# Who issues the DRAM writes of a chunk's regrouping: SP or ScalarE

## The chip, the core and the metric

The kernel runs on one core of a Trainium2 chip. The core has TensorE (PE in the profile), VectorE (DVE), ScalarE (ACT), GpSimd (POOL) and SyncE (SP). SP computes nothing here, it issues transfers; its queue is SPq in the profile, and a transfer that ScalarE issues stands under ACTq. The metric is the device time of one execution in microseconds (us).

## The reference

Attention over pooled keys, then two gated networks, one after the other. Cut to what matters:

```python
kv_pool = kv.reshape(B, H // 4, 4, W // 4, 4, C).mean(axis=(2, 4))   # B 2, H 384, W 32, C 128
k = v = kv_pool.reshape(B, -1, C) @ w_sr                             # 768 keys
s = (q @ k.transpose(0, 2, 1)) / sqrt(C)                             # 12288 queries a batch
a = exp(s - s.max(-1)); a /= a.sum(-1) + 1e-9
x = (a @ v).reshape(-1, C)                                           # 24576 tokens
h = x @ w1_in;  x = (h * cos(h)) @ w1_out                            # d_ff 2048
h = x @ w2_in;  out = (h * sigmoid(1.702 * h)) @ w2_out
```

Every product of two fp32 matrices that needs it is made of three fp32r matmuls: each operand is split into an upper part (`_hi`, rounded to fp32r) and a lower part (`_lo`, the rest).

## The kernel before

The 24576 queries are 48 chunks of 512 (`CHUNKS`; `CB` = 24 a batch), a chunk is 4 tiles of 128 queries (`SUB`), so there are 192 tiles. The attention fills the first 580 us or so; the two networks, pipelined with each other, fill the rest and are not touched.

A tile goes like this. PE computes its scores against 768 keys (`score`, lines 691 to 693). DVE takes the negated maximum (L1259, `neg_max`), ACT the exponentials (L1038, `exponentials`, into one of two buffers `probs`), DVE turns them by blocks of 32x32 (L1271, `turn`, which counts up `turned_made`). The tile's block lands in `turned[b][n]`, the chunk's buffer, n = chunk modulo 3 (two buffers `turned`, the third is `turned_last`).

The turned blocks still have to be moved between partitions before PE can use them as the moving operand of the product with the values. That is `regroup(c)`, and the DMA does it, in two ways. Blocks are numbered by the group a of 32 partitions in which they lie. For a = 0 and 1 there are 8 direct transfers from SBUF to SBUF, of 96 KB each (L475). For a = 2 and 3 there are two writes of 384 KB to a DRAM tensor `bounce` (L469), and then, when both have landed (semaphore `bounced`), one read of 768 KB back into `gathered` (L479). ACT (two thirds, L1057) and POOL (one third, L613) then round `gathered` to `probs_t_hi`, POOL subtracts to get the lower part (L601), and PE sums (`sum_upper` L763 and L765, `sum_lower` L775). ACT then copies the sums out (L1064, `store_x1`) and SP writes them to DRAM (L492).

Each engine has one order of instructions, written out by hand in a loop over tile slots s = 0 to 190. In slot s, ACT does the exponentials of tile s + 2 first; `round_probabilities(c, i)` comes in slot 4c + 8 + i (`HI_SLOT` is 8), after the exponentials of tiles 4c + 10 and 4c + 11. In slots with s % 4 == 3 ACT also rounds the queries of a later chunk (L1027, `split_queries`) and stores a chunk's sums (L1064). SP runs over chunks: load the queries of chunk c + 3 (L455), for c < 12 a piece of the second batch's keys (L449), `regroup(c)`, save the inverse sums (L487), save chunk c - 3 (L492). The two loads of raw weights ahead of `regroup(18)` and the ones at c = 31 and 35 are on SP too (L500, L504).

`regroup(c)` begins with waits for `turned_made` (the chunk's four tiles) and, from chunk 3 on, for `values_summed` of chunk c - 3, whose lower parts lie in the same bytes as `gathered`. DVE's `turn` of a chunk's first tile waits for `regrouped` of chunk c - 3, since the direct transfers and the writes read the buffer that it is about to fill.

Of the kernel before, what the change touches and what calls it, by code (L numbers as in the profile page):

```python
# [22 lines left out]
BLK = 32  # L23
# [17 lines left out]
def attention_and_networks(nc, q, kv, w_sr, w1_in, w1_out, w2_in, w2_out, out):  # L41
# [4 lines left out]
    KEYS = (H // R) * (W // R)  # L46
# [388 lines left out]
    with nc.Block() as block:  # L435

        @block.sync
        def _(sp):
# [19 lines left out]
            def regroup(c):  # L458

                b, n = c // CB, c % 3  # L460
                sp.wait_ge(turned_made, (c + 1) * SUB)
                if c >= 3:
                    sp.wait_ge(values_summed, c - 2)
                if c == CB + 1:
                    sp.wait_ge(piece_made, 4)
                dst, src = gathered[b][n], turned[b][n]
                for a in range(DIRECT, GROUPS):
                    at = slice((a - DIRECT) * KEYS, (a - DIRECT + 1) * KEYS)
                    sp.dma_start(  # L469
                        bounce[c][:, :, at].rearrange("f p x -> p f x"),  # L470
                        src[a * BLK:(a + 1) * BLK, :, :, :].rearrange("p f k t -> p f (k t)")
                    ).then_inc(bounced[n], 16)
                for a in range(DIRECT):
                    for f in range(GROUPS):
                        sp.dma_start(flat(dst[f * BLK:(f + 1) * BLK, a]),  # L475
                                     flat(src[a * BLK:(a + 1) * BLK, f])
                                     ).then_inc(regrouped[n], 16)
                sp.wait_ge(bounced[n], BOUNCED * (c // 3 + 1))
                sp.dma_start(dst[:, DIRECT:GROUPS].rearrange("p a k t -> p (a k t)"),  # L479
                             bounce[c].rearrange("f p x -> (f p) x")  # L480
                             ).then_inc(regrouped[n], 16)
# [542 lines left out]
        def _(act):  # L1024
# [35 lines left out]
            def store_x1(c):  # L1060
                act.wait_ge(values_summed, c + 1)
                if c >= 2:
                    act.wait_ge(x1_saved[c % 2], c // 2 * 16)
                nc.scalar.activation(by_tile(x_out[c % 2][:, :], "tokens"),  # L1064
                                     by_tile(x1_ps[c % 2], "groups"), ACT.Copy).then_inc(x1_ready, 1)

            def copy_part(t):

                act.wait_ge(part_pooled, t + 1)
                nc.scalar.activation(pooled_t[:, t * TKEYS:(t + 1) * TKEYS], pool1_ps,  # L1070
                                     ACT.Copy).then_inc(part_copied, 1)
# [57 lines left out]
            for s in range(TILES - 1):  # L1129
                if s + 2 < TILES:  # L1130
                    exponentials(s + 2)
                c, i = divmod(s - HI_SLOT, SUB)
                if c >= 0 and i < (BY_POOL if c < CHUNKS - 2 else PARTS):
                    round_probabilities(c, i)
                if s % SUB == 1:
                    guard_totals(s // SUB)
                if (s + 5) % SUB == 0 and 2 <= (s + 5) // SUB < CHUNKS:
                    split_queries((s + 5) // SUB, q_ps)
                if s >= STORE_SLOT and (s - STORE_SLOT) % SUB == 0:
                    store_x1((s - STORE_SLOT) // SUB)  # L1140
                t, m = divmod(s - POOL_SLOT, POOL_GAP)
                if 0 <= t < HT and m == POOL_SLOTS:
                    copy_part(t)
                if s in KEY_SLOTS:
                    key_piece(KEY_SLOTS[s])
                if (s - SPLIT_SLOT) % SPLIT_GAP == 0:
                    i = (s - SPLIT_SLOT) // SPLIT_GAP
                    if 0 <= i < WEIGHT_PIECES:
                        round_weights(i)
            store_x1(CHUNKS - 4)  # L1150
            nc.scalar.activation(silu_probe[:, :], half_pi[:, :], ACT.Silu)
            round_probabilities(CHUNKS - 2, 0)
# [327 lines left out]
```

## Time and profile before

| what | value |
|---|---|
| time, median of 3 runs | 2680.96 us (2680.41 to 2684.88) |
| the profiled execution, its own time | 2679.44 us |
| its span, first to last instruction | 2677.7 us |
| what lies around the span | 1.7 us |
| attention, from the start | about 580 us |
| span from SP's read back of chunk 0 to that of chunk 47 | 41.38 to 572.93 us |

The page gives busy time of each engine over the whole span (PE 97%), the DMA queues and the chain of work that ended last. Since the attention is a fifth of the span, its limits don't show in the shares of the whole; they are read from stretches of it. All transfers of the attention are on one queue, q1, SP's; q10 is ScalarE's, and holds only two stores at the very end.

### The profile page before, as it was taken

What the parts mean: (1) busy time and instruction counts of PE and PEld (TensorE: products, weight loads), DVE (VectorE), ACT (ScalarE), POOL (GpSimd) and SP (SyncE); (2) the same over time, 40 slices, a digit from 0 to 9 for tenths busy, and PEclk for the clock granted to TensorE, in tenths of its full rate; (3) what the DMA queues carried; (4) which work ended last, traced back from release to release, by engine and by line L of the source; (5) the groups of instructions that cost most, each with busy time, mean ns of one, the idle gap of its engine ahead of it and who ended that gap; (6) DMA issues with size and microseconds to landing.
All of it is one profiled execution on the core that took longest, in us unless ns stands there. A gap on an engine that the chain in (4) does not pass through costs nothing.

```text
span 2677.7 us, 37678 instructions
## 1 busy us (share of the span) xinstructions
PE 2594.7 (97%) x11797; PEld 2139.9 (80%) x11797; DVE 2076.1 (78%) x2264; ACT 1876.6 (70%) x2280; POOL 2172.9 (81%) x1830
## 2 busy tenths in 40 slices
PE   8998888889999999999999999999999999999999
PEld 6777766767888888888888888888888888888887
DVE  7777777777787777777777878787877787877876
ACT  4655666667777777777777777777777777777776
POOL 2776888879888888888888888888888888888873
PEclk9999999989999999999999999999999999999999
DMA  7988888850101101000101010100101000100000
GB/s 245 296 283 283 260 265 267 276 178 9 24 12 23 23 12 24 12 24 12 24 12 24 12 24 12 24 23 12 24 12 24 12 24 12 24 12 24 12 16 12
DMA packets 191147, 193.88 MB, mean 72 GB/s; under 512 B 113457, under 2 KB 138353, under 8 KB 190065
## 3 DMA queue, kind: packets, MB, share of 16 engines
q1 hardware_dynamic: 190032, 193.03, 24.6%
q8 instruction: 30, 0.49, 0.1%
q10 hardware_dynamic: 1056, 0.13, 0.0%
q14 instruction: 29, 0.23, 0.0%
HBM read 92.34 MB, written 63.01 MB: 58 GB/s over the span
## 4 chain that ended last, share of the span: by engine, by line
PE 80%; SPq 10%; DMA 5%; DVE 1%; issue 1%; POOL 1%; ACT 1%; POOLq 0%
PE psum L691 26%; PE psum L692 26%; PE psum L693 26%; SPq L475 7%; DMA gathered<-bounce 3%; SPq L469 1%; POOL g_lo L676 1%; DMA bounce<-turned 1%; DMA bounce<-turned_last 1%; PE psum L763 1%; DVE neg_max L1259 1%; PE psum L765 1%; ACT probs_t_hi L1057 1%; DVE turned L1271 0%; SPq L479 0%
## 5 line engine op out<-in xcount | busy, mean ns | idle before, releaser
L676 POOL TENSOR_TENSOR g_lo<-g,g_hi 128x512 fp32r<-128x512 f32 x768 | 1120.0, 1459 | 67.7 <-ACT g_hi L1174 7.6
L1392 DVE TENSOR_TENSOR g_lo<-g,g_hi 128x1024 fp32r<-128x1024 f32 (+1 forms) x396 | 643.4, 1625 | 433.3 <-ACT g L1169 432.0
L1167 ACT ACTIVATE g_hi<-psum 128x1024 fp32r<-128x1024 f32 (+1 forms) x396 | 397.3, 1003 | 558.8 <-PE psum L693 558.7
L673 POOL CAST g_hi<-g 128x512 fp32r<-128x512 f32 x750 | 565.1, 753 | 229.8 <-DVE g L1383 229.8
L691 PE MATMUL psum<-x_hi,w_lo 128*128 128x512 f32 x1536 | 598.6, 390 | 1.3 <-DVE g L1383 1.3
L691 PE MATMUL psum<-g_hi,w_lo 128*128 128x512 f32 x1536 | 597.9, 389 | 0.8 <-POOL g_lo L676 0.8
L692 PE MATMUL psum<-x_lo,w_hi 128*128 128x512 f32 x1536 | 598.1, 389 | 0.0
L693 PE MATMUL psum<-x_hi,w_hi 128*128 128x512 f32 x1536 | 598.0, 389 | 0.0
L692 PE MATMUL psum<-g_lo,w_hi 128*128 128x512 f32 x1536 | 597.5, 389 | 0.0
L693 PE MATMUL psum<-g_hi,w_hi 128*128 128x512 f32 x1536 | 597.5, 389 | 0.0
L1383 DVE TENSOR_TENSOR g<-psum,g 128x512 f32<-128x512 f32 x768 | 490.0, 677 | 1.9 <-ACT g L1160 1.8
L1365 DVE SCALAR_TENSOR_TENSOR g<-turns,psum 128x1024 f32<-128x1024 int32 x384 | 462.8, 1205 | 4.3 <-ACT turns L1126 4.1
L1160 ACT ACTIVATE g<-g,half_pi 128x1024 f32<-128x1024 f32 x384 | 442.5, 1152 | 5.1 <-DVE g L1365 5.1
L1126 ACT ACTIVATE turns<-psum 128x1024 int32<-128x1024 f32 x384 | 395.1, 1029 | 3.7 <-PE psum L693 3.7
L1169 ACT ACTIVATE g<-psum 128x1024 f32<-128x1024 f32 (+1 forms) x396 | 393.9, 995 | 0.0
L691 PEld LDWEIGHTS psum<-x_hi,w_lo 128*128 128x128 f32 x1536 | 288.5, 188 | 63.4 <-DVE g L1383 2.8
L691 PEld LDWEIGHTS psum<-g_hi,w_lo 128*128 128x128 f32 x1536 | 288.4, 188 | 61.8 <-POOL g_lo L676 1.6
L693 PEld LDWEIGHTS psum<-x_hi,w_hi 128*128 128x128 f32 x1536 | 288.7, 188 | 60.1
L692 PEld LDWEIGHTS psum<-x_lo,w_hi 128*128 128x128 f32 x1536 | 288.7, 188 | 59.7
L693 PEld LDWEIGHTS psum<-g_hi,w_hi 128*128 128x128 f32 x1536 | 288.2, 188 | 60.1
L601 POOL TENSOR_TENSOR probs_t_lo<-gathered,probs_t_hi 128x1024 fp32r<-128x1024 f32 x140 | 333.3, 2404 | 3.2 <-ACT probs_t_hi L1057 0.4
L692 PEld LDWEIGHTS psum<-g_lo,w_hi 128*128 128x128 f32 x1536 | 288.2, 188 | 59.6
(87 smaller groups left out, 2493.0 us busy)
## 6 DMA issues: line engine op xcount, KB each, us to landing
gathered<-bounce SPq DMA_DIRECT2D x48, 768.0 KB, 5.4
bounce<-turned SPq DMA_DIRECT2D x64, 384.0 KB, 6.2
gathered<-turned SPq DMA_DIRECT2D x256, 96.0 KB, 2.8
bounce<-turned_last SPq DMA_DIRECT2D x32, 384.0 KB, 6.2
gathered<-turned_last SPq DMA_DIRECT2D x128, 96.0 KB, 3.1
x_dram<-x_out SPq DMA_DIRECT2D x48, 256.0 KB, 5.1
x_raw<-x_dram SPq DMA_DIRECT2D x48, 256.0 KB, 2.6
x_inv<-inverse_dram SPq DMA_DIRECT2D x48, 256.0 KB, 3.4
```

The lines of the kernel that those rows point to most:

```text
L673: nc.gpsimd.tensor_copy(g1_hi[at][:, t], g1[at][:, t]).then_inc(g1_hi_ready, 1)
L676: nc.gpsimd.tensor_tensor(g1_lo[at][:, t], g1[at][:, t], g1_hi[at][:, t].bitcast(F32), ALU.subtract).then_inc(g1_lo_ready, 1)
L691: nc.tensor.matmul(dst, w_lo, x_hi, start=start, stop=False)
L692: nc.tensor.matmul(dst, w_hi, x_lo, start=False, stop=False)
L693: return nc.tensor.matmul(dst, w_hi, x_hi, start=False, stop=stop)
L1126: nc.scalar.activation(turns[ring(i, p)][:, :], h1[buffer1(i, p)], ACT.Copy, bias=0.25, scale=1.0 / (2 * math.pi)).then_inc(turns_ready, 1)
L1160: nc.scalar.activation(g1[ring(i, p)][:, :], g1[ring(i, p)][:, :], ACT.Sin, bias=half_pi[:, :]).then_inc(cos_ready, 1)
L1167: nc.scalar.activation(g2_hi[ring2(j, p)][:, t], h2[buffer2(j)][:, t], ACT.Silu, scale=GELU)
L1169: nc.scalar.activation(g2[ring2(j, p)][:, t], h2[buffer2(j)][:, t], ACT.Silu, scale=GELU).then_inc(g2_ready, 1)
L1365: nc.vector.scalar_tensor_tensor(g1[ring(i, p)][:, :], turns[ring(i, p)][:, :], -2 * math.pi, h1[buffer1(i, p)], ALU.mult, ALU.add).then_i ...
L1383: nc.vector.tensor_tensor(g1[ring(i, p)][:, t], h1[buffer1(i, p)][:, t], g1[ring(i, p)][:, t], ALU.mult).then_inc(g1_ready, 1)
L1392: nc.vector.tensor_tensor(g2_lo[ring2(j, p)][:, t], g2[ring2(j, p)][:, t], g2_hi[ring2(j, p)][:, t].bitcast(F32), ALU.subtract).then_inc(g ...
```

## The change

The two writes to `bounce` leave `regroup(c)` on SP and become `bounce_groups(c)`, issued by ScalarE. It waits for the chunk's four tiles in `turned_made`, as `regroup` does, and for nothing else. Its place is slot 4c + 3 of ACT's loop, behind the exponentials of tile 4c + 5 and ahead of the query rounding and the store that follow in that slot; for chunk 47 it comes behind the loop, ahead of the store of chunk 44's sums. SP keeps the 8 direct transfers, the wait for `bounced` and the read back, with all its other transfers in the same order. Sizes, buffers and semaphore counts are the same.

```diff
@@ regroup(c), on SP
                 dst, src = gathered[b][n], turned[b][n]
-                for a in range(DIRECT, GROUPS):
-                    at = slice((a - DIRECT) * KEYS, (a - DIRECT + 1) * KEYS)
-                    sp.dma_start(
-                        bounce[c][:, :, at].rearrange("f p x -> p f x"),
-                        src[a * BLK:(a + 1) * BLK, :, :, :].rearrange("p f k t -> p f (k t)")
-                    ).then_inc(bounced[n], 16)
                 for a in range(DIRECT):
@@ on ACT
+            def bounce_groups(c):
+
+                b, n = c // CB, c % 3
+                act.wait_ge(turned_made, (c + 1) * SUB)
+                for a in range(DIRECT, GROUPS):
+                    at = slice((a - DIRECT) * KEYS, (a - DIRECT + 1) * KEYS)
+                    src = turned[b][n][a * BLK:(a + 1) * BLK, :, :, :]
+                    nc.scalar.dma_start(
+                        bounce[c][:, :, at].rearrange("f p x -> p f x"),
+                        src.rearrange("p f k t -> p f (k t)")
+                    ).then_inc(bounced[n], 16)
@@ ACT's loop over slots
                 if s + 2 < TILES:
                     exponentials(s + 2)
+                if s % SUB == SUB - 1:
+                    bounce_groups(s // SUB)
@@ behind the loop
+            bounce_groups(CHUNKS - 1)
             store_x1(CHUNKS - 4)
```

The engines' orders show the move. On SP, at chunk 25 (`turned_1_85` is the chunk's turned buffer, `gathered_1_88` its regrouped one), this stood between the load of queries and the next saves before:

```order
L455 DMA q_blocks<-in_q 128x4x128
L469 DMA bounce<-turned_1_85 32x4x768 x2
L475 DMA gathered_1_88<-turned_1_85 32x768 x8
L479 DMA gathered_1_88<-bounce 128x1536
```

and this stands there now (the line numbers of what follows the removed lines are 6 lower):

```order
L455 DMA q_blocks<-in_q 128x4x128
L469 DMA gathered_1_88<-turned_1_85 32x768 x8
L473 DMA gathered_1_88<-bounce 128x1536
L481 DMA inverse_dram<-inverse_92 4x128
L486 DMA x_dram<-x_out_60 128x512
```

Two issues a chunk are gone from SP, and nothing has changed places with anything else. On ACT, around the end of a chunk in the first batch, with each instruction's semaphores, before:

```order
L1038 ACTIVATE probs_69,total<-psum,neg_max 128x768 [waits turned_made,max_ready]
L1027 ACTIVATE q_hi_65<-psum 128x512 [waits q_transposed]
L1064 ACTIVATE x_out_59<-psum 128x4x4x32 [waits x1_saved0,values_summed]
L1038 ACTIVATE probs_68,total<-psum,neg_max 128x768 [waits turned_made,max_ready]
```

and now:

```order
L1032 ACTIVATE probs_69,total<-psum,neg_max 128x768 [waits turned_made,max_ready]
L1068 DMA bounce<-turned_1_77 32x4x768 [waits turned_made]
L1068 DMA bounce<-turned_1_77 32x4x768
L1021 ACTIVATE q_hi_65<-psum 128x512 [waits q_transposed]
L1058 ACTIVATE x_out_59<-psum 128x4x4x32 [waits x1_saved0,values_summed]
L1032 ACTIVATE probs_68,total<-psum,neg_max 128x768 [waits turned_made,max_ready]
```

The two issues have come between the exponentials of a chunk's second tile and the three instructions that follow them, the last of which is the next tile's exponentials.

## Rows read from the trace of the kernel before

**Rows 1.** The page: DMA share by fortieths of the span, and SP's queue.

```profile
DMA  7988888850101101000101010100101000100000
q1 hardware_dynamic: 190032, 193.03, 24.6%
```

**Rows 2.** Busy time by stretch: us, PE, PEld, DVE, ACT, POOL, granted clock, DMA share, GB/s.

```profile
41.38:165.81 124.43, 114.42 (x630) 95.80 (x630) 92.74 (x123) 75.38 (x144) 87.47 (x44) 0.99 0.92 296
165.81:232.25 66.44, 61.56 (x351) 52.23 (x351) 48.28 (x66) 40.70 (x80) 47.15 (x24) 1.00 0.86 262
248.02:572.93 324.91, 273.89 (x1326) 220.65 (x1327) 229.16 (x306) 204.94 (x385) 260.77 (x138) 0.95 0.87 266
```

**Rows 3.** Waits between 67 and 580 us: total us, times, longest.

```profile
ACT probs_t_hi L1057 <- DMA gathered<-bounce: 124.7, 43, 8.8
POOL probs_t_hi L613 <- DMA gathered<-bounce: 105.9, 41, 8.4
...
PE psum L763 <- ACT probs_t_hi L1057: 50.2, 30, 7.5
```

**Rows 4.** PE's wait for rounded probabilities, in 67:134, 134:201 and 248:573 us.

```profile
PE psum L763 <- ACT probs_t_hi L1057: 5.0, 6, 1.5
```

```profile
PE psum L763 <- ACT probs_t_hi L1057: 4.0, 4, 1.7
```

```profile
PE psum L763 <- ACT probs_t_hi L1057: 36.3, 17, 7.5
```

**Rows 5.** SP's queue in order of time (start us, us), chunks 24 and 25.

```profile
303.41 0.59 SPq L479 DMA_DIRECT2D gathered<-bounce  x1
304.04 0.35 SPq L487 DMA_DIRECT2D inverse_dram<-inverse  x1
304.43 0.36 SPq L492 DMA_DIRECT2D x_dram<-x_out  x1
304.84 0.42 SPq L455 DMA_DIRECT2D q_blocks<-in_q  x1
305.37 1.23 SPq L469 DMA_DIRECT2D bounce<-turned  x2
306.64 7.66 SPq L475 DMA_DIRECT2D gathered<-turned  x8
314.34 0.59 SPq L479 DMA_DIRECT2D gathered<-bounce  x1
...
316.31 1.16 SPq L469 DMA_DIRECT2D bounce<-turned  x2
```

**Rows 6.** The chain of work between 304 and 330 us (start us, us).

```profile
306.64 1.58 SPq L475
308.21 0.04 issue
308.26 2.23 SPq L475
...
310.53 0.59 SPq L475
...
314.34 6.08 DMA gathered<-bounce
320.41 0.02 issue
320.44 1.06 ACT probs_t_hi L1057
```

**Rows 7.** DVE and ACT in order of time around the ends of chunks 24 and 25.

```profile
300.50 0.97 DVE L1271 STREAM_TRANSPOSE turned<-probs 128x768 uint32<-128x768 uint32 x1
...
310.97 0.98 DVE L1271 STREAM_TRANSPOSE turned<-probs 128x768 uint32<-128x768 uint32 x1 [1.50 <-ACT probs L1038]
```

```profile
309.00 1.06 ACT L1057 ACTIVATE probs_t_hi<-gathered 128x1024 fp32r<-128x1024 f32 x1 [3.00 <-DMA gathered<-bounce]
...
313.89 0.91 ACT L1038 ACTIVATE probs<-psum,neg_max 128x768 f32<-128x768 f32 x1 [1.03 <-DVE neg_max L1259]
```

**Rows 8.** Lines 469 and 479: issue ns, and us from issue to landing (min, median, max).

```profile
L469 SPq DMA_DIRECT2D bounce<-turned x64: 326/524/3575, 33.2 to 552.9; - x64
...
DMA to landing us min/median/max: 4.6/6.2/8.9
```

```profile
L479 SPq DMA_DIRECT2D gathered<-bounce x48: 343/583/1432, 41.4 to 572.9; - x48
```

**Rows 9.** The two queues at the end of the span, each issuing two stores.

```profile
2674.24 0.85 SPq L559 DMA_DIRECT2D out<-y_blocks  x2
```

```profile
2674.25 0.93 ACTq L1214 DMA_DIRECT2D out<-y_blocks  x2
```

## The prediction, made before the changed kernel was run

> **What bounds the kernel now.** Only the attention is touched. In the page the DMA engines are 80 to 90% busy in its eight slices and almost idle behind them [rows 1], so I looked at stretches of it next. Between the read backs of chunks 0 and 11 a chunk takes 124.43 / 11 = 11.31 us, from 11 to 17 66.44 / 6 = 11.07, from 18 to 47 324.91 / 29 = 11.20 [rows 2]. PE is busy for 10.40, 10.26 and 9.44 us of these. In the last stretch PE idles 51.0 us in all, and the waits say for what: 36.3 us for rounded probabilities [rows 4]. Between 67 and 580 us it is 50.2, and ACT and POOL, which round, wait 124.7 and 105.9 us for the read back from DRAM [rows 3]. So the regrouping is late, not the arithmetic.
>
> Why it is late stands in SP's queue [rows 5]. From one read back to the next SP is never free: 0.59 + 0.35 + 0.36 + 0.42 for single transfers, 1.23 for the two writes, 7.66 for the 8 direct ones, and some 0.05 between instructions. That is the period, 314.34 - 303.41 = 10.93 us. The 7.66 is not the cost of 8 issues. In the chain the first two last 1.58 and 2.23 us, the later ones 0.59 [rows 6]: the first two hold 3.81 - 1.18 = 2.6 us of stall. They follow the transfers with the most pieces: queries (512 rows of 512 bytes) and two writes of 128 pieces each, while the previous read back is still being moved. I read that as a queue that is full.
>
> The whole is a loop over two chunks. Chunk 24's last tile is turned at 300.50 + 0.97 = 301.47 [rows 7], its read back has landed and ACT rounds at 320.44 [rows 6]: L = 18.97 us. From such a rounding to the turning of the tile behind it, the last of the chunk but one further on, is 309.00 to 311.95, 2.95 us [rows 7] (ACT issues in order, so no exponentials pass a rounding that waits). L + 2.95 = 21.92, two periods of 10.96. What shortens L by x shortens the period by x / 2, until something else holds.
>
> **The change, part by part.**
>
> SP loses the two write issues: 1.23 us a chunk [rows 5].
>
> SP's stall goes, or most of it. Without the writes there are 256 pieces fewer in front of the direct transfers, of about 1028 (read back 128, inverse 4, sums 128, queries 512, writes 256). Bounds: 0 if what stops SP is the DMA engines themselves, 2.6 us if it is the count in its own queue. I take most of it, because the stall ends while the engines stay busy, and the later issues run at an even 0.59. SP then needs 10.93 - 1.23 - 2.6 = 7.1 us a chunk and is no bound any more.
>
> The writes start earlier. Now they are issued at 316.31 for a chunk that was turned at 311.95. On ACT they come behind the exponentials that begin at 313.89, so at about 314.8 [rows 5, 7], 1.5 us earlier, in a queue of their own instead of behind the read back and the queries. Nothing shows that landing; the nearest rows are 4.6 to 8.9 us, median 6.2 [rows 8]. I take the median and keep 4.6.
>
> SP gets a new place to wait: its 8 direct issues end about 5.1 us (8 x 0.64) behind the turning, the writes land later, so SP now stands in the wait for `bounced` with the inverse, the sums, the next queries and the next direct transfers behind it. New L: 2.85 to ACT's issue, 0.5 to the second one, 6.2 to landing, 6.1 for the read back [rows 6] = 15.65. With 2.95 that is 18.6 over two chunks, 9.3 us a period (8.5 with 4.6). This is below or at what PE needs (9.44 + the 14.7 / 29 = 0.5 us of idle that has other causes = 9.95), so the wait on SP costs nothing unless it grows by about 1.3 us.
>
> ACT gains two issues a chunk. Bounds: 326 to 3575 ns each on SP [rows 8]; on ACT only the two at the end, 0.93 together while SP issued two in 0.85 [rows 9]. I take 1.0 us a chunk. ACT is busy 204.94 / 29 = 7.1 us a chunk [rows 2], so 8.1 of 9.95 fits. But it delays query rounding, store and the next exponentials, and at a pace without slack some of it shows: 0.07 us a chunk, 3 us in all (0 to 0.3 a chunk).
>
> The DMA engines carry the same bytes. They are 92% busy in the first stretch and 87% in the last [rows 2]: 0.87 x 11.20 = 9.7 us a chunk. Part of that is waiting inside transfers that come one by one, so it can shrink; in the first stretch, where the second batch's keys are loaded as well, there is less room.
>
> The Trainium skill speaks against this change here: DMA: Bandwidth & Descriptors, "Issuing engines are not separate DMA queues", says that transfers from different engines share the same 16 DMA engines, and that issuing from several saves only the issuing sequencer's time, usually small. The rows show 3.8 us of SP's period in writes and stall, which is not small; what the rule alone would give is the first rival.
>
> **The sum.** All of PE's waits for probabilities: 50.2 us. Kept: half of the 9.0 us between 67 and 201 us, where DMA has little room (4.5), and half of the longest wait, 7.5 us, behind the 1 MB weight loads that stay ahead of the regrouping on SP (3.7). Added: ACT's 3. Gain 50.2 - 4.5 - 3.7 - 3 = 39 us. Against the profiled execution's own 2679.44 us that is 2640.4; it stands 1.5 below the median of the runs, so against that 2642. The networks and what lies around the span are unchanged. What is late next is PE itself, with POOL close behind (260.77 / 29 = 9.0 us a chunk [rows 2]). The far end of the gain is all of PE's idle time in the three stretches, 10.0 + 4.9 + 51.0 = 66 us, 2615.
>
> **The rivals.**
>
> Only the issues go. The 2.6 us of stall come from busy engines and stay, in the direct transfers; SP's 1.23 us go, 0.6 a period in the two-chunk loop, 47 x 0.6 = 28 us, 2653. For it: the stall lasts as long as the read back moves. Against: there is less in the queue then. This is what the Trainium skill's rule above comes to.
>
> DMA bound. If the engines hold no more than the 92% of the first stretch, the first 18 chunks gain nothing, and the others stop at 9.7 / 0.92 = 10.6 us: 29 x 0.6 = 17 us, 2664 (2656 to 2672). For it: both queues meet in the same engines, and the read back can now be delayed by the next chunk's writes, which stood behind it before. Against: the direct issues at 0.59 us each leave gaps that the writes can fill.
>
> Nothing moves. If SP's stall only becomes a wait for `bounced`, because the writes land when they landed before, L stays 18.97 and so does the period: 2681, within 5. For it: the same bytes. Against: the writes' earlier issue.
>
> ACT is held, slower. If an issue on ACT stalls as SP's do, the 2.6 + 1.2 us move to ACT: 7.1 + 3.8 = 10.9 us busy, with dependent waits of at least another 1.4 a chunk (the exponentials wait for maxima), a period of 12.3 or 1.1 above the 11.20: 47 x 1.1 = 52 us, 2733. It decides from an issue time of (10.9 - 7.1 - 1.0) / 2 = 1.4 us each. Against: ACT's queue holds only 256 pieces, and at the end of the span two queues issuing at once did not slow each other [rows 9].
> The skill gives this rival a mechanism: Perfetto Trace Analysis, "DMA Instruction — HWDGE (DVE, Sync)", says that the descriptor generator is locked by one sequencer at a time, and that the profiled issue holds this wait. Rows 9 show at most 0.08 us of it.
>
> **How the numbers follow.** Forecast 0.45 (2642, its own range 2616 to 2656); only the issues 0.15; DMA bound 0.20; nothing moves 0.08; ACT held 0.09; better than 2616 0.03. The range reaches over the forecast, the issues alone and the DMA-bound case, 2616 to 2672, and leaves out 0.2. A measurement of this kernel can tell about 0.2% (5.4 us) from no change. Faster: 0.45 + 0.15 + 0.20 + 0.03 = 0.83; within: 0.08; slower: 0.09.
>
> **What would show it.** Right, if the read backs of chunks 18 and 47 lie about 290 us apart instead of 325; if the first direct issues last 0.6 us; if SP's waits show the read back waiting for `bounce`; if ACTq's two issues take 0.5 us each; if PE's wait at L763 falls under 15 us. DMA bound, if DMA share is at 95% and the read back lands later than 6 us. ACT held, if ACTq issues last over 1.4 us and DVE's wait for `probs` grows. The forecast is wrong if the writes take much over 7 us to land in their own queue, since every further microsecond adds 0.5 to the loop.

## The result, and the profile after

The changed kernel takes 2649.74 us (median of 4 runs, 2646.09 to 2651.34) against 2680.68 before (2678.97 to 2684.88). The ratio is 0.9882, with a 95% interval of 0.9867 to 0.9897: 31 us faster. It had been predicted 8 us faster than that, 2642, with a range of 2616 to 2672.

The profiled execution has a span of 2647.8 us, 29.9 less than before. All of that lies in the attention. SP's read back of chunk 47 is issued at 541.97 instead of 572.93 us, 30.96 earlier. Busy time by stretch between the read backs of chunks 0, 11, 17, and 18 to 47, columns as in [rows 2]:

```profile
40.56:159.47 118.91, 111.81 (x619) 93.25 (x618) 90.67 (x123) 75.83 (x144) 86.02 (x43) 0.99 0.96 307
159.47:221.25 61.78, 61.22 (x354) 52.28 (x353) 47.61 (x64) 41.23 (x77) 47.56 (x24) 1.00 0.93 288
234.88:541.97 307.09, 269.59 (x1327) 218.42 (x1325) 228.28 (x311) 206.20 (x385) 256.25 (x138) 0.95 0.92 282
```

The first stretch is 5.5 us shorter than in [rows 2], the second 4.7, the last 17.8; another 2.1 come between chunks 17 and 18 and 0.8 before chunk 0. A chunk now takes 10.81, 10.30 and 10.59 us. In the second stretch PE is busy for 61.22 of 61.78 us, so there it is the bound. In the last it still idles 37.5 us (51.0 before). The DMA share (the column before the last) has risen from 0.92, 0.86 and 0.87 to 0.96, 0.93 and 0.92.

What PE waits for between 67 and 580 us has changed. Before, it was 50.2 us for rounded probabilities from ScalarE [rows 3], 11.2 for their lower parts, and under 5 for the rest:

```profile
PE psum L775 <- POOL probs_t_lo L601: 11.2, 15, 1.4
```

After (us in all, times, longest):

```profile
PE psum L757 <- ACT probs_t_hi L1051: 20.5, 12, 6.7
PE psum L787 <- DMA q_blocks<-in_q: 12.8, 12, 2.1
PE psum L769 <- POOL probs_t_lo L595: 7.0, 9, 1.6
```

L757 is the old L763: 30 us of its wait are gone. L769 is the old L775. The wait for queries (L787) is new: they now land a median of 6.3 us behind their issue, where it was 5.6. They stay in SP's queue while ScalarE's writes use the same DMA engines; that this is the cause was not tried by itself. PE's busy time in the three stretches fell too, from 449.9 to 442.6 us.

SP's queue at chunk 25, against [rows 5] (start us, us). The rows of L469, the eight direct issues, come from narrow looks; together they last 8.45 us from 299.62:

```profile
299.08 0.43 SPq L455 DMA_DIRECT2D q_blocks<-in_q  x1
299.62 1.26 SPq L469 DMA_DIRECT2D gathered<-turned  x2
300.92 2.55 SPq L469 DMA_DIRECT2D gathered<-turned  x1
303.52 2.00 SPq L469 DMA_DIRECT2D gathered<-turned  x1
...
308.12 0.59 SPq L473 DMA_DIRECT2D gathered<-bounce  x1
```

The two issues of 1.23 us are gone, but the stall is not. In this chunk it sits in the third and fourth direct issue, 2.55 and 2.00 us, and not in the first and second [rows 6]. Over all 48 chunks it has spread: the eight direct issues now last 0.76 to 1.04 us on average, each with a median near 0.6, where before the first took 1.21, the second 1.80 and the others 0.62 to 0.84. ACT in the same time:

```profile
300.14 0.90 ACT L1032 ACTIVATE probs<-psum,neg_max 128x768 f32<-128x768 f32 x1 [1.44 <-DVE neg_max L1268]
300.15 0.87 ACTq L1068 DMA_DIRECT2D bounce<-turned  x2
300.95 0.19 ACT L1032 ACTIVATION_READ_ACCUMULATOR probs<-psum,neg_max 128x1 f32 x1
301.07 0.60 ACT L1021 ACTIVATE q_hi<-psum 128x512 fp32r<-128x512 f32 x1
```

The two issues begin with the exponentials that stand ahead of them in the program, not behind them, and are over when these are: ScalarE issues while it computes. The first issue begins within 0.1 us of these exponentials in 47 of the 48 chunks. Over the whole kernel the issues take a median of 0.40 us each (the row is of the chunks in `turned`; those in `turned_last` have a median of 395 ns):

```profile
L1068 ACTq DMA_DIRECT2D bounce<-turned x64: 309/399/1532, 34.2 to 526.3; - x64
...
DMA to landing us min/median/max: 3.4/6.3/9.9
```

And SP's own waits, of which the first was 2.3 us in 3 chunks before:

```profile
SPq L473 <- DMA bounce<-turned: 17.4, 14, 2.8
...
SPq L473 <- DMA bounce<-turned_last: 4.0, 7, 0.9
```

### The profile page after: what moved, and what is told of

It reads as the page before. It is cut to its first block, busy times and chain, and to the rows that moved or that the text cites. A ratio compares the mean times of both kernels' runs of the same rounds, so it can differ in the third digit from the quotient of the medians.

```text
span 2647.8 us, 37678 instructions
## 1 busy us (share of the span) xinstructions
PE 2587.5 (98%) x11797; PEld 2136.3 (81%) x11797; DVE 2068.8 (78%) x2264; ACT 1880.8 (71%) x2280; POOL 2173.4 (82%) x1830
## 4 chain that ended last, share of the span: by engine, by line
PE 85%; DMA 7%; SPq 3%; POOL 3%; DVE 1%; issue 1%; ACT 0%; POOLq 0%
PE psum L685 27%; PE psum L687 27%; PE psum L686 27%; SPq L469 2%; DMA q_blocks<-in_q 2%; DMA bounce<-turned 2%; POOL probs_t_lo L595 1%; DMA gathered<-bounce 1%; POOL g_lo L670 1%; PE psum L757 1%; PE psum L759 1%; PE psum L769 1%; DVE neg_max L1268 1%; DMA bounce<-turned_last 1%; PE psum L787 1%
## 5 line engine op out<-in xcount | busy, mean ns | idle before, releaser
L667 POOL CAST g_hi<-g 128x512 fp32r<-128x512 f32 x750 | 558.4, 745 | 226.5 <-DVE g L1392 226.5
L1169 ACT ACTIVATE g<-g,half_pi 128x1024 f32<-128x1024 f32 x384 | 442.6, 1153 | 4.0 <-DVE g L1374 4.0
L595 POOL TENSOR_TENSOR probs_t_lo<-gathered,probs_t_hi 128x1024 fp32r<-128x1024 f32 x140 | 334.3, 2410 | 14.8 <-ACT probs_t_hi L1051 13.2
```

Source lines behind the costliest of these rows:

```text
L667: nc.gpsimd.tensor_copy(g1_hi[at][:, t], g1[at][:, t]).then_inc(g1_hi_ready, 1)
L1169: nc.scalar.activation(g1[ring(i, p)][:, :], g1[ring(i, p)][:, :], ACT.Sin, bias=half_pi[:, :]).then_inc(cos_ready, 1)
```

## The experiments

What had to be explained: the stall that was expected to go stayed, and yet most of the gain came. Four numbers are followed through all runs. They are worked out from each kernel's trace: the time between the read backs of chunks 18 and 47 (29 chunks), its length per chunk, the stall in SP's direct issues per chunk (what each is longer than 0.6 us, mean over 48 chunks; e10 has six such issues on SP instead of eight), and the time. The kernel before was measured anew beside each group of runs, with medians from 2679.3 to 2681.9, and each ratio below goes by its own; so two changed kernels a few us apart are compared by their ratios.

| kernel | time, us | 18 to 47 | a chunk | stall |
|---|---|---|---|---|
| before | 2680.7 | 324.9 | 11.20 | 2.57 |
| the change | 2649.7 | 307.1 | 10.59 | 2.41 |
| e1 queries in 2 KB rows | 2645.3 | 302.4 | 10.43 | 2.21 |
| e2 queries issued by ScalarE | 2681.0 | 319.4 | 11.01 | 2.22 |
| e3 before, small issues on ScalarE | 2683.6 | 328.1 | 11.31 | 2.64 |
| e4 one write each | 2654.2 | 306.3 | 10.56 | 1.86 |
| e5 before, short writes | 2613.3 | 271.5 | 9.36 | 0.22 |
| e6 change, small issues on SP | 2684.5 | 328.6 | 11.33 | 1.02 |
| e7 writes a slot later | 2667.8 | 306.6 | 10.57 | 2.22 |
| e8 writes ahead of the exponentials | 2643.1 | 300.7 | 10.37 | 2.12 |
| e9 e8 with e1 | 2644.4 | 301.1 | 10.38 | 2.21 |
| e10 e8, two direct ones on ScalarE | 2643.8 | 299.3 | 10.32 | 2.52 |
| e11 before, queries behind | 2712.3 | 338.1 | 11.66 | 2.66 |
| e12 change, short writes | 2609.9 | 272.8 | 9.41 | 0.37 |

### What the stall is: e1, e5 and e11

Queries as 128 rows of 2 KB, on the changed kernel:

```diff
-    q_rows = q.rearrange("b (n s p) c -> (b n) p s c", s=SUB, p=P)
-    out_chunks = out.rearrange("(n m a) (j c) -> n j a m c", m=TOK // BLK, a=BLK, c=BLK)
+    q_rows = q.rearrange("b (n p s) c -> (b n) p s c", s=SUB, p=P)
+    out_chunks = out.rearrange("(n u a v) (j c) -> n j a v u c", u=P // BLK, a=BLK, v=SUB, c=BLK)
...
```

The rest of the edit puts the stores of `out` in the same order.

> The changed kernel (2649.7 us), with one thing more: a chunk's queries are loaded as 128 rows of 2 KB instead of 512 rows of 512 bytes (the tokens of a chunk are dealt to its tiles in another order, and the stores of the output put them back). The bytes are the same. In the changed kernel SP still stalls about 2.4 us a chunk in its direct issues, only later in the row of eight (in the fourth to sixth, where before it was the first two). Theory count: SP's queue stops when it holds about 1024 pieces, one per transfer and DMA engine for the completion counted in. 384 pieces fewer: the stall goes, under 0.5 us a chunk, the read backs of chunks 18 and 47 come under 300 us apart (307.1 now), time 2630 to 2642. Theory engines: the stall is the backlog of busy DMA engines, whatever its pieces. The 512 rows take 0.86 us of all engines, 128 rows of 2 KB 0.67: 0.2 us a chunk less, stall still about 2.2 us, time 2644 to 2650.

2645.27 us, ratio to before 0.9868 (0.9852 to 0.9885), so 4.5 below the changed kernel's median, with intervals that overlap. With 384 pieces fewer the stall is 2.21 us instead of 2.41, a difference that can't be told from none, since the stall varies by 1.1 us from chunk to chunk. The count theory is out by its own number (under 0.5); its limit of 1024 pieces is one that no run shows.

The kernel before, writes of the same 128 pieces each but a sixth of the bytes. The read back is as long as ever and always takes what chunk 0 wrote, so what the kernel leaves out is five sixths of the writes, and its output is not the reference's:

```diff
                 for a in range(DIRECT, GROUPS):
-                    at = slice((a - DIRECT) * KEYS, (a - DIRECT + 1) * KEYS)
+                    k = KT if c == 0 else 1
+                    at = slice((a - DIRECT) * KEYS, (a - DIRECT) * KEYS + k * P)
...
-                        src[a * BLK:(a + 1) * BLK, :, :, :].rearrange("p f k t -> p f (k t)")
+                        src[a * BLK:(a + 1) * BLK, :, 0:k, :].rearrange("p f k t -> p f (k t)")
...
-                             bounce[c].rearrange("f p x -> (f p) x")
+                             bounce[0].rearrange("f p x -> (f p) x")
```

> The kernel before, with the two writes still on SP and still of 128 pieces each, but from chunk 1 on only 128 of the 768 columns are written; the read back is as long as ever and always reads what chunk 0 wrote, so the output is not the reference's. It takes away five sixths of the writes' bytes (640 KB, about 1.6 us of all DMA engines a chunk) and none of their pieces. Theory count (SP stalls when too many pieces stand in its queue): the stall of 2.6 us a chunk in the direct issues stays, what is gained is only the shorter landing, 2665 to 2680. Theory backlog (SP stalls behind the bytes that the engines have not moved yet, the writes' above all): the stall falls to about 1 us or less, 2635 to 2655, and more than the changed kernel gained if it goes altogether.

2613.34 us, ratio 0.9755 (0.9738 to 0.9771), and the stall is gone: 0.22 us. All issues are still on SP. Its queue in one chunk (start us, us):

```profile
316.59 0.92 SPq L470 DMA_DIRECT2D bounce<-turned  x2
317.55 4.96 SPq L476 DMA_DIRECT2D gathered<-turned  x8
322.57 0.57 SPq L480 DMA_DIRECT2D gathered<-bounce  x1
```

Eight issues in 4.96 us, where [rows 5] have 7.66. The number of pieces is the same in both kernels (the page counts 190032 packets on SP's queue in each). So what stops SP in its direct issues goes with the bytes of the two writes, or the time that the DMA engines take for them, and not with the number of pieces. PE is then nearly always busy (stretch of chunks 18 to 47):

```profile
230.10:501.50 271.40, 256.70 (x1319) 208.88 (x1318) 227.38 (x309) 203.72 (x381) 253.81 (x136) 0.99 0.85 248
```

It is busy for 256.70 of 271.40 us, at a granted clock of 0.99 (0.95 before and after the change). The run shortens the writes' landing too (median 4.5 us instead of 6.2) and reads the same DRAM rows each time, so the 67 us are the price of the bytes in all, not of the stall alone.

The queries moved behind the direct transfers, all on SP:

```diff
-                if c + 3 < CHUNKS:
-                    load_queries(c + 3)
                 if c < HT * SUB:
...
@@ regroup(c), on SP
                                      ).then_inc(regrouped[n], 16)
+                if c + 3 < CHUNKS:
+                    load_queries(c + 3)
                 sp.wait_ge(bounced[n], BOUNCED * (c // 3 + 1))
```

> The kernel before, all issues on SP, with one thing moved: the queries of chunk c + 3 are loaded behind the eight direct transfers of chunk c instead of ahead of its writes. Number of issues, bytes and engines are the same; the writes no longer stand behind 512 rows of queries. Theory SP's time: the same, within 5 us of before, 2675 to 2685. Theory order in the queue (the writes' place behind the queries costs): the writes land about 1 us earlier, but nothing waits for them on SP, 2670 to 2680. The queries come about 8 us later; if that is too late PE waits for them, 2690 to 2740.

2712.27 us, ratio 1.0126 (1.0106 to 1.0146): the queries come too late, as the last case said, though they land a median of 3.0 us behind their issue instead of 5.6.

```profile
PE psum L793 <- DMA q_blocks<-in_q: 77.6, 39, 9.8
```

For the stall it says one thing. Without the 512 rows of queries ahead of the writes it is 2.66 us and still sits in the first two direct issues (1.48 and 1.92 us on average). The queries' place ahead of the writes is not its cause.

### Whose time was gained: e6 and e3

Two small issues given back to SP, in front of the direct ones of the changed kernel (the DRAM tensor `spare`, a semaphore and a wait ahead of the loop are not shown):

```diff
                 dst, src = gathered[b][n], turned[b][n]
+                for k in range(2):
+                    sp.dma_start(spare[c, k].rearrange("f p x -> p f x"),
+                                 row_mean[0:BLK, :].rearrange("p (f x) -> p f x", f=GROUPS)
+                                 ).then_inc(spare_saved, 16)
```

> The changed kernel, with two issues given back to SP in the place of the writes: 128 pieces of 32 bytes each from a constant tile to a spare DRAM tensor, which nothing waits for. It gives SP its issue time back (about 1 us a chunk) without bytes. Theory issue time (what was gained is the 1.23 us of SP's queue, half of it a period): the gain is lost, 2670 to 2682. Theory own queue (what was gained is that the writes no longer stand behind the read back and the queries in SP's queue, and start earlier): most stays, 2650 to 2662. From the loop over two chunks an SP that is always busy should show 0.5 us a chunk at least: 2672.

2684.53 us, ratio 1.0017 (1.0007 to 1.0027): the whole gain is lost, and a little more. The time is 2.5 us above the range of the theory that had foretold this. Nothing waits for these transfers, they carry 4 KB each, and the writes stay in ScalarE's queue and start as early: over chunks 18 to 46 the first write is issued 2.7 us behind the turning, against 2.5 in the changed kernel and 4.8 in the kernel before. So the writes' own queue and earlier start are worth little by themselves, and what the change gained was the room in SP's queue. What the run gives back is a little more than issue time, though: it is also 256 pieces of 32 bytes ahead of the direct transfers, for which the DMA engines need time. In e3 these pieces cost nothing in ScalarE's queue; in SP's queue they were not tried apart from their issues. The stall moves: it falls to 1.02 us in the direct issues, since the small ones in front of them take it. Their min, median and max in ns, then the first and last start:

```profile
L470 SPq DMA_DIRECT2D spare<-row_mean x96: 325/644/5157, 33.1 to 574.5; - x96
```

Over chunks 18 to 47 the two take 2.28 us a chunk and the direct ones 5.77, together 8.05. Before the change the two writes took 1.20 and the direct ones 7.39, together 8.59. The rest of the 11.33 is single transfers, which have grown from 1.84 to 2.54 us, and SP's waits and gaps.

The same two small issues on ScalarE, in the kernel before (`small_writes` holds the two issues of e6):

```diff
                 if s + 2 < TILES:
                     exponentials(s + 2)
+                if s % SUB == SUB - 1:
+                    small_writes(s // SUB)
```

> The kernel before, with two more issues a chunk on ScalarE at the very place where the changed kernel has its writes: 128 pieces of 32 bytes each from a constant tile to a spare DRAM tensor; nothing reads them. SP is as before. It measures ScalarE's cost of two issues by itself. Prediction's term: 3 us in all (0 to 0.3 us a chunk, up to 14), 2681 to 2690. Rival, from the changed kernel's trace where an issue on ScalarE begins together with the exponentials ahead of it (0.87 us of issues beside 0.90 of exponentials): nothing, within 3 us of before. If ScalarE were held by SP's stalls: over 2700.

2683.58 us, ratio 1.0007 (0.9997 to 1.0018), that is 2 us with an interval from -1 to 5. Two issues a chunk on ScalarE cost nothing that can be told from no change; on SP the same two cost 35 us (e6), there in the changed kernel, here in the kernel before.

### The place and the dose: e7, e8 and e4

```diff
                 if s + 2 < TILES:
                     exponentials(s + 2)
-                if s % SUB == SUB - 1:
-                    bounce_groups(s // SUB)
+                if s % SUB == 0 and s > 0:
+                    bounce_groups(s // SUB - 1)
```

> The changed kernel, with ScalarE's two issues one slot later, behind the query rounding, the store and the exponentials of tile 4c + 6, about 2.0 us later. Loop theory (L sets the period, half of what is added to it shows): 1.0 us a chunk, 47 us, 2690 to 2700. If SP's queue sets it and the writes have slack: the changed kernel's SP waited 21 us in all for the writes in 21 of 48 chunks, so most of the 2 us shows as wait on SP but partly takes the place of stall: 2660 to 2680. If DMA engines alone set it: within 5 us of 2650.

2667.75 us, ratio 0.9955 (0.9941 to 0.9970): 18 us above the changed kernel, not the 47 of the loop theory. From chunk 18 to 47 it is no longer at all (306.6 against 307.1); the loss is in the stretches before. SP's wait for the writes has grown from 21.4 to 58.7 us, in 30 chunks. In chunks 18 to 47 it took the place of issue time: SP's issues last 8.84 us a chunk instead of 9.57. The waits in all:

```profile
SPq L473 <- DMA bounce<-turned: 38.1, 21, 5.6
SPq L473 <- DMA bounce<-turned_last: 20.6, 9, 4.6
```

The other way round:

```diff
-                if s + 2 < TILES:
-                    exponentials(s + 2)
                 if s % SUB == SUB - 1:
                     bounce_groups(s // SUB)
+                if s + 2 < TILES:
+                    exponentials(s + 2)
```

> The changed kernel, with the two issues ahead of the exponentials in their slot instead of behind them. These wait for the same turned tile anyway and then, mostly, for DVE's maximum (ScalarE idle 1.44 us in the chunk of chunk 24), so the writes go out up to 1.5 us earlier. Loop theory: L shorter by 1.0 to 1.5, 0.5 to 0.7 us a chunk in the chunks that wait for probabilities, 12 to 33 us: 2620 to 2638. If the queue on SP or the DMA engines set the period: within 6 us of 2650. Rival: the 0.87 us of issues now stand in front of the exponentials and delay them; then 2650 to 2665.

2643.13 us, ratio 0.9871 (0.9850 to 0.9892). The median is 6.6 us below the changed kernel's, less than the 12 to 33 of the loop theory; by the ratios it is 3 us, and the intervals overlap, so no gain is shown. Yet the writes start 2.5 us earlier: over chunks 18 to 46 the first is issued 0.05 us behind the turning instead of 2.5.

Half the change; the first of the two writes stays in `regroup` on SP:

```diff
@@ bounce_groups(c), on ACT
-                for a in range(DIRECT, GROUPS):
+                for a in range(GROUPS - 1, GROUPS):
@@ regroup(c), on SP
+                for a in range(DIRECT, GROUPS - 1):
+                    at = slice((a - DIRECT) * KEYS, (a - DIRECT + 1) * KEYS)
+                    sp.dma_start(
+                        bounce[c][:, :, at].rearrange("f p x -> p f x"),
...
```

> Half the change: SP issues the first of the two writes, ScalarE the second, each where it stands in the kernel before and in the changed one. Theory issues (a period falls by half of what SP sheds): SP sheds 0.6 us and 144 pieces, half the gain: 2665, 2660 to 2670. Theory landing (the read back has to wait for both writes, so the later of the two decides): most of the gain is lost, 2670 to 2680. Theory engines only: between 2650 and 2660, since the same bytes move and they are not held back much.

2654.18 us, ratio 0.9898 (0.9880 to 0.9917): half of the issues moved bring 26.5 of the 31 us, and the intervals of half and whole overlap. Both theories that had the gain follow the issues or the later landing missed it; the third, which let the bytes hold the rest back, gave 2650 to 2660. In chunks 18 to 47 it is even (306.3 against 307.1), with a stall of 1.86 us instead of 2.41. There the write that is left on SP takes 1.00 us a chunk. When it leaves as well, the direct issues last 0.65 us more and SP's waits and gaps 0.30 more, which takes it back.

### How far it can be carried: e2, e9, e10 and e12

Query loads on ScalarE as well:

```diff
                 if (s + 5) % SUB == 0 and 2 <= (s + 5) // SUB < CHUNKS:
                     split_queries((s + 5) // SUB, q_ps)
+                    if (s + 5) // SUB + 1 < CHUNKS:
+                        load_queries((s + 5) // SUB + 1)
...
```

SP's own `load_queries(c + 3)` in its loop is gone.

> The changed kernel, with the query loads of chunks 3 to 47 issued by ScalarE too, right behind the rounding of the queries whose buffer they refill. Bytes and pieces are the same, 512 pieces a chunk leave SP's queue for ScalarE's. Theory count: SP's queue holds 528 pieces fewer and its direct issues do not stall; SP needs 10.6 - 2.4 - 0.5 = 7.7 us a chunk and waits for the writes instead; the stretch from chunk 18 to 47 falls under 300 us, time 2628 to 2642. Theory engines: the stall of 2.4 us stays on SP or comes to ScalarE's issues; SP's issue of 0.46 us and the earlier queries (PE waited 12.8 us for them in the changed kernel) are the only gain, 2640 to 2648. If an issue on ScalarE costs it its full 0.4 us, DVE's wait for probs grows by 15 us or more over the 45 chunks.

2681.04 us, ratio 1.0007 (0.9997 to 1.0018): all of the gain is lost, against both theories. They had not asked what the queries stand behind in the new queue. The writes are issued just ahead of them:

```profile
308.72 0.91 ACTq L1070 DMA_DIRECT2D bounce<-turned_last  x2
309.51 0.19 ACT L1034 ACTIVATION_READ_ACCUMULATOR probs<-psum,neg_max 128x1 f32 x1
309.68 0.60 ACT L1019 ACTIVATE q_hi<-psum 128x512 fp32r<-128x512 f32 x1
309.70 1.21 ACTq L1023 DMA_DIRECT2D q_blocks<-in_q  x1
311.01 0.60 ACT L1060 ACTIVATE x_out<-psum 128x512 f32<-128x512 f32 x1 [0.73 <-issue]
```

The queries land 7.1 us behind their issue (6.3 in the changed kernel, 5.6 in the kernel before), and PE waits for them. That the writes ahead of them are what delays them is how I read it; no run has them in that queue without the writes.

```profile
PE psum L785 <- DMA q_blocks<-in_q: 58.0, 36, 8.8
```

Here ScalarE is held too. The third issue takes a median of 1.61 us and the store behind it waits for it, 46.0 us in 41 chunks (`ACT x_out L1060 <- issue` in the waits). That is the rival "ACT is held", one issue further than it was put.

The two small gains together, the edits of e8 and e1:

```diff
+                if s % SUB == SUB - 1:
+                    bounce_groups(s // SUB)
                 if s + 2 < TILES:
                     exponentials(s + 2)
...
+    q_rows = q.rearrange("b (n p s) c -> (b n) p s c", s=SUB, p=P)
```

> The changed kernel with two edits that each gained a little: ScalarE's two writes ahead of the exponentials of their slot (2643.1 alone, 6.6 us) and the queries loaded as 128 rows of 2 KB (2645.3 alone, 4.5 us). If they act on different things (the writes' start, the bytes in small rows) they add: 2636 to 2641. If both only use up the same slack: 2641 to 2645.

2644.36 us, ratio 0.9854 (0.9836 to 0.9873). By the medians they don't add (2643.1 and 2645.3 alone). By the ratios, 0.9871 and 0.9868 alone against 0.9882 of the change, they would, and the intervals are as wide as the gains: it stays undecided.

Two of the eight direct transfers to ScalarE, behind the exponentials of the slot, on top of e8:

```diff
+                for f in range(GROUPS // 2, GROUPS):
+                    nc.scalar.dma_start(flat(gathered[b][n][f * BLK:(f + 1) * BLK, 1]),
+                                        flat(turned[b][n][BLK:2 * BLK, f])
+                                        ).then_inc(regrouped[n], 16)
```

> The changed kernel with the writes ahead of the exponentials (2643.1), and two of SP's eight direct transfers issued by ScalarE, right behind these exponentials. It takes 1.2 us of issues off SP, as the change did, but adds to ScalarE's queue a third and fourth issue while the writes are being moved. Theory SP's time (period falls when SP sheds issues): another 10 to 20 us, 2623 to 2635. Theory backlog (an issue stalls behind the writes on whatever engine it is; with the queries on ScalarE its third issue took 1.2 to 1.7 us and held the store behind it): ScalarE is held by 1 to 2 us a chunk, 2645 to 2675.

2643.78 us, ratio 0.9862 (0.9846 to 0.9879), the same as e8. SP sheds another 1.2 us of issues a chunk and nothing comes of it. ScalarE's issues now stall too, while those left on SP still do:

```profile
300.57 0.90 ACT L1032 ACTIVATE probs<-psum,neg_max 128x768 f32<-128x768 f32 x1 [1.15 <-DVE neg_max L1283]
300.63 3.06 ACTq L1081 DMA_DIRECT2D gathered<-turned  x2
301.37 0.19 ACT L1032 ACTIVATION_READ_ACCUMULATOR probs<-psum,neg_max 128x1 f32 x1
303.74 0.60 ACT L1021 ACTIVATE q_hi<-psum 128x512 fp32r<-128x512 f32 x1 [2.18 <-issue]
```

Two issues behind the writes last 3.06 us here (median 1.06 each over the kernel), and the next instruction waits 2.18 us for them. The two engines stall together. SP's second direct issue ends at 301.08 us and ScalarE's first at 301.16, SP's third (2.35 us) at 303.47 and ScalarE's second (2.49 us) at 303.69. Each of the 53 issues of ScalarE over 1 us overlaps one of SP over 0.9 us, and 34 end within 0.25 us of such a one.

Last, the short writes of e5 with the two issues on ScalarE:

```diff
@@ bounce_groups(c), on ACT
+                    k = KT if c == 0 else 1
+                    at = slice((a - DIRECT) * KEYS, (a - DIRECT) * KEYS + k * P)
+                    src = turned[b][n][a * BLK:(a + 1) * BLK, :, 0:k, :]
...
@@ regroup(c), on SP
-                             bounce[c].rearrange("f p x -> (f p) x")
+                             bounce[0].rearrange("f p x -> (f p) x")
```

> The changed kernel with the shortened writes of the run before (from chunk 1 on 128 of 768 columns are written, the read back always reads what chunk 0 wrote, so the output is not the reference's): the same 640 KB a chunk less, but the two issues on ScalarE. With the writes on SP the shortening took 67 us off the kernel before, and the stall in the direct issues fell from 2.6 to 0.2 us a chunk. Theory one cause (both the change and the shortening only relieve SP's queue, and PE is the bound once that is done): with the stall gone, SP's two issues no longer matter, 2605 to 2614, within 8 us of the 2613.3 with the writes on SP. Theory two costs (SP's issue time and the bytes cost apart from each other): the gains add, 2613 - 31 = 2582, at least below 2600.

2609.86 us, ratio 0.9737 (0.9721 to 0.9753), 3.5 below e5, with intervals that overlap: without the bytes, the issues hardly matter. With the stall gone SP's queue has room, PE is busy for 272.65 of 285.00 us between 215 and 500 us, and SP's 1 us of issues disappears in the room. The run can't tell one cause from two: both kernels stand near what PE allows. PE is busy for 2575.6 us of e12's whole span, so the 2582 of the theory of two costs would leave it some 6 us idle in all.

## Why the prediction was right, and where it was not

**The bound** was read rightly. SP was never free at the chunks shown [rows 5], and e6 shows that what is given back to it costs the whole gain.

**SP's stall goes, or most of it.** This step failed. 2.6 us were read as a queue full of pieces and taken out of SP's 10.93; the changed kernel has 2.41. The lower bound of that term, "0 if what stops SP is the DMA engines themselves", was the true one, for a reason that e5 shows: the bytes of the writes. The rows that could have told it were there. The stall began with the read back still being moved and two writes just issued, and the DMA share was 0.87 to 0.92 [rows 2]; "the stall ends while the engines stay busy" was read as speaking against the engines, while it can as well say that their backlog had become short enough.

**The term that followed from it** was too large by just that. SP was to need 7.1 us a chunk. Added up over chunks 18 to 47 its issues take 9.57 us a chunk, with another 1.02 of waits and gaps. The direct ones are 7.31 of it (7.39 before), the writes' 1.20 are gone, the single transfers have grown from 1.84 to 2.26 and waits and gaps from 0.77 to 1.02: 1.20 + 0.08 - 0.42 - 0.25 = 0.61, by which the period fell.

**The loop over two chunks** held before, and half of what was expected of it came. From the turning of a chunk's last tile to ACT's rounding it took 19.4 us on average over chunks 18 to 45, and 17.5 in the changed kernel, so L fell by 1.9 us and not by the 3.3 of 18.97 to 15.65. Chunk 25, of which the rows are, is one of the shortest (they reach from 14.1 to 23.1): turned at 298.57, read back at 308.12, rounded at 313.36, which is 14.8 us.

```profile
297.60 0.97 DVE L1280 STREAM_TRANSPOSE turned<-probs 128x768 uint32<-128x768 uint32 x1
```

```profile
313.36 1.06 ACT L1051 ACTIVATE probs_t_hi<-gathered 128x1024 fp32r<-128x1024 f32 x1 [1.03 <-DMA gathered<-bounce]
```

With the 2.95 us behind it the average closes a loop of (17.5 + 2.95) / 2 = 10.2 us a period, a little under the 10.59 measured; before it was 11.2, the period itself. So the loop binds some chunks and no longer all: ACT waits for the read back in 24 of them instead of 43, and for DVE's maxima, which wait for PE, 107.1 us instead of 65.8. What would be "late next" was named as PE, at 9.95, and the kernel stopped at 10.6 before it. I put that down to SP and the DMA engines, from e5 and e6. e7 and e8 agree that the writes' start counts for little now: 2 us more cost 18 us instead of 47, and 2.5 us less gained nothing that is clear of noise, where 1.5 were to gain 12 to 33.

**The writes** start at 300.15 in chunk 25, 1.6 us behind the turning, since ScalarE issues beside its exponentials; over chunks 18 to 46 it is 2.5 us, where 2.85 was taken. They land after a median of 6.3 us where 6.2 was taken. SP waits 21.4 us in all for them; what that costs was not tried.

**ScalarE's cost** was taken as 3 us and measured as 2 with an interval that holds zero (e3), for two issues. For a third and fourth it would have been wrong (e2, e10).

**The sum** came near partly by luck. Of 50.2 us of PE's waits, 42 were to go before ScalarE's 3; 29.7 went. Against that came 12.8 us for queries, which no term had. Two things that the prediction did not have made up for much of it: 4.2 us less for lower parts, and 7.2 us less of PE's busy time. Together that is 29.7 - 12.8 + 4.2 + 7.2 = 28.3 of the 29.9 us by which the span fell. In the stretch of chunks 18 to 47 the waits for probabilities were 36.3 us [rows 4]; 18.3, half of them, stayed. The prediction's sign for this, the read backs of 18 and 47 some 290 us apart and the wait at L763 under 15 us, did not come (307.1 and 20.5).

**The rivals.** "Only the issues go", 2653, has the mechanism: the stall stays. The period falls by 0.61 where it said 0.6, but this agreement is luck. The 0.6 was half of 1.23 in the loop, and the 0.61 is what is left when single transfers, waits and gaps have taken their part. It was given 0.15. "DMA bound" put its mark at a share of 95%; the first stretch is at 96 and the last at 92, and e5 and e12 show the time 36 and 40 us lower still when the engines have fewer bytes to move. The two look like one thing seen from SP and from the engines. The Trainium skill's rule, that issuing from another engine saves the sequencer's time and nothing of the DMA engines' (DMA: Bandwidth & Descriptors, "Issuing engines are not separate DMA queues"), is borne out: e10 shows that more of it saves nothing. The same section of the Trainium skill calls that time usually small "relative to the DMA itself", and here it is: 0.6 us an issue against 6.2 to landing. It does not say that it is of no account, as the prediction took it to, and in a queue that sets the pace 1.2 us a chunk were worth 31 us. The lock that another page of the Trainium skill describes (Perfetto Trace Analysis, "DMA Instruction — HWDGE (DVE, Sync)") is hardly seen in the change: with SP issuing all the time ScalarE's issues take 0.40 us. Nor does a stalled SP hold it for as long as it stalls. In e7 both issues of ScalarE lie within one stalled issue of SP and last as long as elsewhere:

```profile
376.81 4.65 SPq L469 DMA_DIRECT2D gathered<-turned  x1
377.07 0.81 ACTq L1068 DMA_DIRECT2D bounce<-turned  x2
```

So the 3.06 us of e10 are not explained by a lock that SP holds while it stalls; that both engines' stalls end together there speaks for something that they share and that drains.

**Open.** What exactly fills up when SP stalls. It follows the bytes of the writes and not the number of pieces (e1, e5), and it strikes the issues of both engines (e10). What it is was not tried, nor how much of the 31 us is issue time alone (e6 gives back small pieces with it).

## What to carry to other kernels

When an issuing queue is never free, split its row into issue time and stall before costing what leaves it: here the part above the usual issue time went with the bytes in flight and stayed with them, wherever they were issued. Moving two issues a chunk to an engine that computes is then worth only their plain issue time, but on the queue that sets the pace that was 1.2%, and half of the move brought about as much. Be wary of putting a transfer that somebody waits for behind large ones in the new queue (e2), and of a third issue in a row behind 768 KB of writes, since from there the computing engine stalled too (e2, e10). Read a queue over all chunks before believing one of them: the chunk shown here was among the shortest.

## What the runs showed of the hardware that was not expected

- ScalarE's issue of a transfer runs beside the activation ahead of it: 300.15 against 300.14 us, 0.87 beside 0.90 us. Two issues a chunk cost the kernel 2 us, with an interval from -1 to 5 (e3).
- An issue's length follows the bytes of earlier transfers more than their pieces: the stall of the direct ones fell from 2.57 to 0.22 us a chunk when the writes lost 640 KB (e5), and from 2.41 to 2.21 when the queries lost 384 of their 512 pieces (e1).
- The stall is met by whichever issue comes next, small or large: in e6 two transfers of 4 KB took 2.28 us a chunk, in e10 ScalarE's direct ones had a median of 1.06 us each and 3.06 for the two shown.
- A stalled issue of SP (4.65 us in e7) did not hold two issues of ScalarE within it (0.81 us together), but where both stalled (e10) 34 of ScalarE's 53 long issues ended within 0.25 us of a long one of SP.
- The granted clock of TensorE was 0.95 over chunks 18 to 47 before and after the change, with PE idle 51.0 and 37.5 us there, and 0.99 in e5 with 14.7 us idle.
